# A 16-head masked attention with split operands: a new order of SyncE's queue, and scores eleven slots ahead

## The reference

```
# 1. attention over (2, 8) heads of 768 x 64, masked by a 6-bit hash
mask   = bucket(q @ proj > 0) == bucket(k @ proj > 0)
scores = where(mask, q @ k.T / 8, -1e9)
attn   = exp(scores - max(scores)) / (sum + 1e-9);  x = attn @ v
# 2. x as (2, 768, 512): a causal convolution of 5 taps gives the gate
y = (sigmoid(conv(x)) * (x @ w_val)) @ w_out
# 3. Fourier mixing, norm, feed-forward
u = y + real(fft(fft(y, seq), channels));  un = norm(u)
out = u + relu(un @ w_ch1) @ w_ch2
```

## Time and profile before

| | |
|---|---|
| median of 3 runs | 784.6 us (783.83 to 794.24) |
| the profiled execution, and its span | 781.99 us, span 780.1 us |
| mean granted TensorE clock | 0.954 of full speed |
| TensorE busy | 701.6 us (90%) |
| VectorE busy | 418.7 us (54%) |
| GpSimd busy | 381.9 us (49%) |
| ScalarE busy | 278.4 us (36%) |

### The profile page before, as it was taken

The page is one execution under the profiler, slowest core; times in us unless marked ns, Lnnn a source line. Parts: engine busy times, 40 slices in busy tenths (PEclk is TensorE's granted clock), DMA queues, the critical chain, the costliest instruction groups (busy, mean ns, idle before and its releaser), DMA issues.

```text
span 780.1 us, 10303 instructions
## 1 busy us (share of the span) xinstructions
PE 701.6 (90%) x3696; PEld 647.9 (83%) x3696; DVE 418.7 (54%) x573; ACT 278.4 (36%) x424; POOL 381.9 (49%) x283
## 2 busy tenths in 40 slices
PE   2588889788888879878999999999999999999998
PEld 1388888787878778877989899998999999999897
DVE  3365578778888787797485467942122221212112
ACT  2146564455465454565352444211111111111110
POOL 1047778767878787788286697488100000000000
PEclk9589999999999999997999999999999999999999
DMA  9443645544544635111012112323010000001001
GB/s 246 116 123 98 155 118 139 129 113 107 144 113 112 158 106 129 50 31 42 17 50 61 41 42 75 88 85 95 11 40 0 0 28 13 0 0 41 1 0 41
DMA packets 33608, 57.67 MB, mean 74 GB/s; under 512 B 9232, under 2 KB 15632, under 8 KB 33568
## 3 DMA queue, kind: packets, MB, share of 16 engines
q1 hardware_dynamic: 33568, 57.14, 27.8%
HBM read 31.81 MB, written 3.24 MB: 45 GB/s over the span
## 4 chain that ended last, share of the span: by engine, by line
PE 71%; DVE 17%; DMA 4%; SPq 2%; issue 2%; POOL 2%; ACT 0%; DVEq 0%; POOLq 0%
PE psum L1057 63%; DVE max_col L808 4%; DVE neg_parts L818 2%; DMA a2k<-hash_bits 2%; DVE gate L862 1%; DVE qk_lo L794 1%; POOL p_lo L524 1%; DMA flag_dram<-a2q 1%; PE psum L1133 1%; DVE neg_rest L820 1%; PE psum L1138 1%; PE psum L1139 1%; PE psum L1135 1%; PE psum L1136 1%; DVE gate L859 1%
## 5 line engine op out<-in xcount | busy, mean ns | idle before, releaser
L524 POOL TENSOR_TENSOR p_lo<-probs,p_hi 128x768 fp32r<-128x768 f32 x96 | 190.2, 1996 | 66.4 <-ACT probs L647 65.1
L1028 DVE SCALAR_TENSOR_TENSOR h_lo<-psum,h_hi 128x384 fp32r<-128x384 f32 x64 | 35.7, 558 | 182.7 <-ACT h_hi L769 182.7
L808 DVE TENSOR_REDUCE max_col<-psum 128x1 f32<-128x768 f32 x96 | 91.6, 954 | 76.7 <-PE psum L1057 76.1
L644 ACT ACTIVATE p_hi<-psum 128x768 fp32r<-128x768 f32 x96 | 78.0, 813 | 104.6 <-PE psum L1057 103.0
L769 ACT ACTIVATE h_hi<-psum 128x384 fp32r<-128x384 f32 x64 | 31.5, 492 | 214.5 <-PE psum L1057 214.5
L1057 PE MATMUL psum<-a1k,a1q 128*128 128x384 f32 x192 | 74.2, 386 | 26.8 <-DMA a2k<-hash_bits 17.8
L1057 PE MATMUL psum<-unt_hi,w_hi 128*128 (+1 forms) x256 | 86.9, 339 | 0.0
L1057 PE MATMUL psum<-unt_lo,w_hi 128*128 (+1 forms) x256 | 86.3, 337 | 0.0
L1057 PE MATMUL psum<-unt_hi,w_lo 128*128 (+1 forms) x256 | 85.9, 336 | 0.0
L647 ACT ACTIVATE probs<-psum 128x768 f32<-128x768 f32 x96 | 77.3, 805 | 0.0
L1057 PE MATMUL psum<-w_lo,h_hi 128*128 128x512 f32 x192 | 75.9, 395 | 0.0
(11 more groups left out here) (124 smaller groups left out, 1561.6 us busy)
## 6 DMA issues: line engine op xcount, KB each, us to landing
stg_w<-in_w SPq DMA_DIRECT2D x32, 256.0 KB, 2.6
qk_raw<-in_qk SPq DMA_DIRECT2D x16, 384.0 KB, 5.1
a1k<-qk_hi SPq DMA_DIRECT2D x32, 192.0 KB, 5.1
flag_b<-flag_dram SPq DMA_DIRECT2D x16, 384.0 KB, 3.9
v_raw<-in_v SPq DMA_DIRECT2D x16, 192.0 KB, 3.0
a1q<-qk_hi SPq DMA_DIRECT2D x16, 192.0 KB, 4.7
a2q<-qk_hi SPq DMA_DIRECT2D x16, 192.0 KB, 5.3
a1q<-qk_lo SPq DMA_DIRECT2D x16, 192.0 KB, 5.0
```

The lines of the kernel that those rows point to most:

```text
L524: pool.tensor_tensor(p_lo[i % PBUF][:, :], probs[i % PBUF][:, :], bits(p_hi[i % PHBUF][:, 0:S]), ALU.subtract).then_inc(p_lo_ready, 1)
L644: act.activation(halves(p_hi[i % PHBUF][:, 0:S]), ring[ring_st(i) % 2], ACT.Exp, scale=SCALE).then_inc(p_hi_ready, 1)
L808: dve.tensor_reduce(max_col[:, i % T:i % T + 1], s_ps, AX.XY, ALU.max).then_inc(max_done, 1)
L1028: dve.scalar_tensor_tensor(h_lo[:, half], psum[:, j % 2, 0:HALF], 0.0, bits(h_hi[:, half]), ALU.max, ALU.subtract).then_inc(h_lo_ready, 1)
```

## The change

- `S_LEAD` goes from 10 to 11 and `FIRST` from -20 to -21; the hash, its bits and the loads that belong to it move by a slot, and so does `max_parts` (g modulo 6 from 1 to 0). `turn_max` stays.
- SyncE's loop is reordered. `spread_flag` is cut into `store_flag` (g modulo 6 is 5) and `spread_flag` (1), `spread_rec` into `store_rec` (4) and `spread_rec` (0, for the head before). `load_v` moves from two heads ahead to one, and q and k are loaded at g modulo 12 = 2.
- `scale_x` runs almost a head later, and the taps of the convolution four slots later. At the end of attention four taps move from ahead of the gate products to behind `lo_x(1, c)`, and the last reciprocals ahead of the gate products.
- V is loaded in place, in pieces of 64 columns, into tiles of 128 columns whose other half holds ones; `hi_v` and `lo_v` then work on all 128 columns.
- Units can be weighed unsplit, with two matmuls of probs and v. `SPLIT` lists the tiles of a head that are split; it lists all six.

```diff
-ST_LEAD, S_LEAD = 2, 10
-FIRST = -20
+ST_LEAD, S_LEAD = 2, 11
+FIRST = -21
+
+SPLIT = (0, 1, 2, 3, 4, 5)
+
+def splits_until(i):
+    return i // T * len(SPLIT) + sum(j < i % T for j in SPLIT)
+
+def is_split(i):
+    return i % T in SPLIT
 def hash_slot(pair):
-    return 2 * T * pair - 14
+    return 2 * T * pair - 15
...
             def load_v(n):
+                par = n % 2
                 if n >= 2:
-                    sp.wait_ge(vh_ready, n - 1)
                     sp.wait_ge(vl_ready, n - 1)
-                sp.dma_start(v_raw[n % 2][:, :], v[n // H, n % H, :, :].rearrange("(p t) d -> p (t d)", t=T)).then_inc(v_loaded[n % 2], 16)
+                    sp.wait_ge(pv_done, T * (n - 1))
+                sp.dma_start(tiles(v1[par][:, :])[:, :, par * D:(par + 1) * D],
+                             v[n // H, n % H, :, :].rearrange("(p t) d -> p t d", t=T)).then_inc(v_loaded[par], 16)
...
+            def store_flag(n):
+                sp.wait_ge(max_rows, n + 1)
+                sp.dma_start(flag_dram[n:n + 1, :], bits(a2q[n % SETS][FLAG:FLAG + 1, :])).then_inc(flag_stored[n % 2], 16)
+
             def spread_flag(n):
-                sp.wait_ge(max_rows, n + 1)
-                sp.dma_start(flag_dram[n:n + 1, :], bits(a2q[n % SETS][FLAG:FLAG + 1, :])).then_inc(flag_stored, 16)
...
-            for g in range(FIRST, UNITS + T):
+            for g in range(FIRST, UNITS + 2 * T + 3):
                 pair, n = g // (2 * T), g // T
-                if g % (2 * T) == 10 and 0 <= pair + 3 < NPAIR and pair + 3 >= RAWS // 2:
-                    load_qk(2 * (pair + 3))
-                    load_qk(2 * (pair + 3) + 1)
+                if g % T == 1 and 1 <= n <= NH:
+                    fold_den(n - 1)
+                    if n + 1 < NH:
+                        load_v(n + 1)
+                if g % T == 4 and 1 <= n <= NH:
+                    store_rec(n - 1)
+                if g % T == 0 and 2 <= n <= NH + 1:
+                    spread_rec(n - 2)
                 if g % (2 * T) == 6 and 0 <= pair + 2 < NPAIR:
                     stack(2 * (pair + 2))
                 if g % (2 * T) == 10 and 0 <= pair + 2 < NPAIR:
                     stack(2 * (pair + 2) + 1)
-                if g % (2 * T) == 0 and 0 <= pair + 1 < NPAIR:
-                    stack_bits(pair + 1)
-                if g % T == 2:
-                    if 2 <= n + 2 < NH:
-                        load_v(n + 2)
-                        load_wa(n + 2)
-                    if 1 <= n <= NH:
-                        spread_rec(n - 1)
-                if g % T == 4 and 0 <= n + 1 < NH:
-                    spread_flag(n + 1)
-                if g % T == 1 and 1 <= n <= NH:
-                    fold_den(n - 1)
+                if g % (2 * T) == 11 and 0 <= pair + 2 < NPAIR:
+                    stack_bits(pair + 2)
+                if g % T == 5 and 0 <= n + 1 < NH:
+                    store_flag(n + 1)
+                if g % T == 1 and 0 <= n < NH:
+                    spread_flag(n)
+                if g % (2 * T) == 2 and 2 <= pair + 2 < NPAIR:
+                    load_qk(2 * (pair + 2))
+                    load_qk(2 * (pair + 2) + 1)
+                if g % T == 3 and 2 <= n + 2 < NH:
+                    load_wa(n + 2)
...
-                if g % T == 3 and 0 <= n + 1 < NH:
+                if g % T == 4 and 0 <= n + 1 < NH:
                     lo_v(n + 1)
-                if g % T == 1 and 0 <= n < NH:
+                if g % T == 5 and 0 <= n < NH:
                     split_weights(n)
-                if g % T == 4 and 1 <= n <= NH:
-                    scale_x(n - 1)
-                    pool.wait_ge(x_ready, n)
+                if g % T == 2 and 2 <= n <= NH + 1:
+                    scale_x(n - 2)
+                    pool.wait_ge(x_ready, n - 1)
...
-                if g % T == 1 and 0 <= n + 1 < NH:
+                if g % T == 0 and 0 <= n + 1 < NH:
                     max_parts(n + 1)
-                if g % (2 * T) == 10 and 0 <= pair + 2 < NPAIR:
+                if g % (2 * T) == 9 and 0 <= pair + 2 < NPAIR:
                     sign_bits(pair + 2)
-                if g % (2 * T) == 5 and 0 <= pair + 2 < NPAIR:
+                if g % (2 * T) == 4 and 0 <= pair + 2 < NPAIR:
                     lo_qk(2 * (pair + 2))
-                if g % (2 * T) == 7 and 0 <= pair + 2 < NPAIR:
+                if g % (2 * T) == 6 and 0 <= pair + 2 < NPAIR:
                     lo_qk(2 * (pair + 2) + 1)
-                if g % T == 2 and 1 <= n:
+                if g % T == 3 and 1 <= n:
                     reciprocals(n - 1)
-                slot, tap = (g - 18) // (2 * T), (g - 18) % (2 * T) // 2
-                if 0 <= slot < NPAIR - 1 and (g - 18) % 2 == 0 and tap < KCONV:
+                slot, tap = (g - 22) // (2 * T), (g - 22) % (2 * T) // 2
+                if 0 <= slot and (g - 22) % 2 == 0 and tap < KCONV:
                     convolve(slot, tap)
...
-                if g % (2 * T) == 10 and 0 <= pair + 2 < NPAIR:
+                if g % (2 * T) == 9 and 0 <= pair + 2 < NPAIR:
                     hash_pair(pair + 2)
```

More of the change, by code:

```diff
@@ L57, in hashes_until @@
 def hashes_until(g):
-    return min(NPAIR, max(0, (g + 14) // (2 * T) + 1))
+    return min(NPAIR, max(0, (g + 15) // (2 * T) + 1))
 def sts_until(g):
@@ L203, in build @@
         assert top[0] <= g_at
-        vh = [at(g_at, "vh0", T * P, F32R), after("vh1", T * P, F32R)]
-        vl = [after(f"vl{i}", T * P, F32R) for i in range(2)]
+        vh = [at(g_at, "vh0", len(SPLIT) * P, F32R), after("vh1", len(SPLIT) * P, F32R)]
+        vl = [after(f"vl{i}", len(SPLIT) * P, F32R) for i in range(2)]
         probs_at = top[0]
[L207 to L210, removed]
+        probs = [at(probs_at, "probs0", PCOLS)]
+        probs += [after(f"probs{i}", PCOLS) for i in range(1, PBUF)]
+        p_lo = [at(probs_at, "p_lo0", PCOLS, F32R)]
+        p_lo += [after(f"p_lo{i}", PCOLS, F32R) for i in range(1, PBUF)]
+        top[0] = max(top[0], gv_at)
         sums = [after(f"sums{i}", S) for i in range(2)]
@@ L285, in build @@
         max_rows = sem("max_rows")
[L286 removed]
+        flag_stored = [sem(f"flag_stored{i}") for i in range(2)]
         flag_loaded = [sem(f"flag_loaded{i}") for i in range(2)]
@@ L490, in _ @@
                 pool.memset(bits(p_hi[i][:, S + 1:PCOLS]), 0.0).then_inc(consts_ready, 1)
+            for i in range(PBUF):
+                pool.memset(probs[i][:, S:S + 1], 1.0).then_inc(consts_ready, 1)
+                pool.memset(probs[i][:, S + 1:PCOLS], 0.0).then_inc(consts_ready, 1)
             for par in range(2):
-                own, rest = (slice(D, P), slice(0, D)) if par else (slice(0, D), slice(D, P))
-                pool.memset(bits(tiles(vh[par][:, :])[:, :, rest]), 1.0).then_inc(consts_ready, 1)
-                pool.memset(bits(tiles(vl[par][:, :])[:, :, rest]), 0.0).then_inc(consts_ready, 1)
+                rest = slice(0, D) if par else slice(D, P)
+                pool.memset(tiles(v1[par][:, :])[:, :, rest], 1.0).then_inc(consts_ready, 1)
             pool.wait_ge(consts_ready, CONSTS)
@@ L631, in hi_v @@
                     act.wait_ge(pv_done, T * (n - 1))
-                act.copy(tiles(vh[par][:, :])[:, :, par * D:(par + 1) * D], tiles(v_raw[par][:, :])).then_inc(vh_ready, 1)
+                act.copy(vh[par][:, :].rearrange("p (t d) -> p t d", d=P), split_tiles(v1[par][:, :])).then_inc(vh_ready, 1)
             def rows_of_max(n):
@@ L987, in lo_un @@
                 dve.tensor_tensor(part(unt_lo), tile(psum[:, 6 + t % 2, :]), bits(part(unt_hi)), ALU.subtract).then_inc(unt_lo_ready, 1)
-            for tap in range(3, KCONV):
-                convolve(NPAIR - 2, tap)
+            reciprocals(NH - 1)
             dve.wait_ge(x_ready, NH - 1)
             gate_values(0, 0)
-            reciprocals(NH - 1)
             gate_values(0, 1)
@@ L997, in _ @@
                 lo_x(1, c)
+            for tap in range(1, KCONV):
+                convolve(NPAIR - 2, tap)
             for tap in range(KCONV):
@@ L1125, in weigh_v @@
                 par, w = n % 2, slice(j * P, (j + 1) * P)
-                hi, lo = p_hi[i % PHBUF], p_lo[i % PBUF]
                 first, last = psum[:, PV_BANK, 0:HALF], psum[:, PV_BANK + 1, 0:HALF + 2]
+                start, stop = j == 0, j == T - 1
                 if j == 0:
-                    pe.wait_ge(vl_ready, n + 1)
+                    pe.wait_ge(v_loaded[par], 16 * (n // 2 + 1))
+                    if SPLIT:
+                        pe.wait_ge(vl_ready, n + 1)
                     if n > 0:
@@ L1131, in weigh_v @@
                         pe.wait_ge(sums_ready, n)
-                pe.wait_ge(p_hi_ready, i + 1)
-                pe.matmul(first, vh[par][:, w], hi[:, 0:HALF], start=j == 0, stop=False)
-                pe.matmul(last, vh[par][:, w], hi[:, HALF:PCOLS], start=j == 0, stop=False)
+                if not is_split(i):
+                    pe.wait_ge(probs_ready, i + 1)
```

(17 more changed lines are left out.)

57 lines of the change are left out of this document (33 added, 24 removed).

## The result

The changed kernel takes 828.7 us at the median of four runs, against 784.2 for the one before: a ratio of 1.056 (95% interval 1.050 to 1.0615). The forecast was 788 with 810 as upper end, so the prediction was wrong, on the far side of its range.

A forecast was written before the change was run, and what follows sets the result against it. No engine full: 48.7 us of waits and clock loss in five pairs bound the attention. Attention +1, prologue +1.5, end +1 sum to +3.5 on 782.0, so 785.5; median forecast 788, eight in ten 764 to 810.

The forecast's parts named there:

- SPLIT changes nothing, waits move from the turn to the scores: Attention: every unit keeps six matmuls; the max chain's wait moves from the turn to the scores, growing by 1.8 to 2.0.
- That is 9.8 against 9.7, +0.1 a pair: Attention, per pair of heads: waits and clock loss cost 9.8 us instead of 9.7, +1 us over seven pairs.
- The 1.3 us a pair that the sum kept for the clock: Attention, per pair of heads: loss to a lower clock behind long waits, kept at 1.3 us as before.
- it lies under the chain's 3.6 [...], so I cost it at nothing: Hash bits, second slot of a pair: TensorE's wait of 2.2 us is covered by the max chain's 3.6, cost nothing.
- Wait 3.6 and 4.5 in the chain's slots: Scores wait for the maximum queued behind VectorE's max chain: 3.6 us in one head of a pair, 4.5 in the other.
- the first rival's cheap chain: VectorE's max chain takes 2.0 us because GpSimd, not held for rec_b, is idle: -29 us, 759; chance 17%.
- GpSimd: rec_b's wait goes, the wider lo_v is covered: GpSimd in attention: 25.3 us of waiting for rec_b go and pay for lo_v's +0.85 a head, 14 us in all.
- The V load in pieces of 256 B: V load one head ahead: landing was 3.0 us, some 8 available; even doubled to 6 it is covered, so nothing.
- Prologue +1.5: Before the first PV: one more scores-only slot costs 0.7 to 2.70 us, taken as +1.5.
- End of attention +1: Last slots, where GpSimd sets the pace: scale_x, lo_v and last weight split less rec_b's wait, +1 us, between -3 and +4.
- the moved taps: Four taps behind the gates (6.2 us) run into an idle 3.92; the 2.3 left over are covered by matmuls.
- the third: SyncE's queue: store_rec behind reciprocals delays stack and bits 2 us a pair beyond cover: +14, 802; chance 12%.

The follow-up runs named there:

- e1: The changed kernel with the weight split back at slot 1 of a head on GpSimd: 780.5 us, ratio 0.9926 to the kernel before.
- e7: e1 with the flag stored and spread in one step at slot 4, ahead of the hash bits in SyncE's queue: 811.3 us, ratio 1.0331.
- e4: e1 with max_col in two halves and the max chain behind the next slot's maximum (slot 1 instead of 0): 801.7 us, ratio 1.0175.
- e5: e1 with scores ten slots ahead again, and max chain, hash, q/k splits and bits on their old slots: 812.1 us, ratio 1.0361.
- e8: e1 with hi_v and lo_v again on the own 64 columns of each tile only: four runs of 797.7 to 811.0 us.
- e10: e1 with convolution taps and second qk_lo moved away from the max chain, and hi_v and lo_v on the own 64 columns only: 780.9 us, ratio 0.9972.
- e11: e1 with one more wait of SyncE, for the p_lo of slot 5, ahead of each weight load: 803.1 us, ratio 1.0251.
- e2: The changed kernel, split still at slot 5, with the weight load asked for at slot 1 of the head after: 795.4 us, ratio 1.0109.

## Why the prediction was wrong, step by step

- **SPLIT changes nothing, waits move from the turn to the scores:** right. neg_parts 23.1 to 2.8 us, max_col 25.6.
- **"That is 9.8 against 9.7, +0.1 a pair": the step that failed.** It was (236.9 - 163.2) / 5 = 14.7 us a pair. The sum had a term for each engine's edits, but for SyncE's queue it began at sign_bits' end and listed store_rec, stack and bits. `load_wa` stands ahead of store_rec in that list, and its wait for a split that was moved from slot 1 to 5 was not read. The bits' wait at m1 came out at up to 7.1 us instead of 2.2. With that term gone (e1) it is 203.8 us for the five pairs, 8.1 a pair. The 1.3 us a pair that the sum kept for the clock were too few as well: after the bits' wait in slot 37 the granted clock was 0.50 from 202.4 to 207 us, some 2.3 us of work lost in that one place.
- **"it lies under the chain's 3.6 [...], so I cost it at nothing":** wrong as a habit. It nearly held in e1, where the bits' waits are 1.4 to 1.7 us. But e7's 3.4 us more in the queue took the cover away, and they passed through to TensorE, six times.
- **Wait 3.6 and 4.5 in the chain's slots:** the size is near. In e1 slots 37 and 38 (m1, m2) took 4.16 and 4.10, 3.3 over two free ones, and slots 42 to 44 had 4.4 over three. But the judgement that this order makes it worse than the order before fell with e4 and e5. Its estimate took one length for the chain, 4.35. In e1 the chain takes 4.8 us where it begins in m0 and 2.25 in m6, as GpSimd's operations fall. In the changed kernel it takes 2.6 and 2.1 to 2.6 from slot 24 to 72: the first rival's cheap chain (2.0) was nearly there, and gave nothing while the bits were late.
- **GpSimd: rec_b's wait goes, the wider lo_v is covered:** wrong in the changed kernel (32.0 us of waiting), since rec_dram is behind the same stop; in e1 the wait in all is 10.6. The wider lo_v costs nothing; the narrow one does (e8, e10). The V load in pieces of 256 B landed in 3.1 us, before 3.0. The line rate that the Trainium skill ("DMA: Bandwidth & Descriptors", Specifications) puts at 512 B and more made no difference that this trace shows.
- **Prologue +1.5:** it was +4.8, and +3.9 in e1, both beyond the 2.70 that I took as the most. The slot itself cost that price: e1's first PV comes 2.7 us behind that of e5, which has one such slot fewer. The other 1.2 us of e1, which e5 has too, are not explained.
- **End of attention +1:** the slots from 72 on lost 9.1 us, with the stand, and 5.2 in e1 without it, so the +1 was too small and its bound of +4 too; 4.0 of the 5.2 are in slots 72 to 84. Behind PV it was 0.3, so the moved taps were covered as said.
- **Rivals:** the third, that SyncE's new order only changes what it stands for, had the right place, but named reciprocals instead of the split and allowed +14.

## What to carry to other kernels

When an instruction moves, look for every queue that waits for it, and list the waits of an in-order queue in the order in which they are met. Here a wait at slot 3 for work at slot 5, for a weight load that was wanted only two heads later, cost 23 to 25 us alone (e11) and 47 to 50 with the late split itself, through the bits issued behind it. Cost a wait in a queue by what stands behind it, not by what it guards. And take the largest wait away before judging the rest: the same move of taps gave 14 us with the queue free and nothing with it blocked.

## What was not expected of the hardware

Less work on an engine made the kernel slower (e8: GpSimd's lo_v 0.85 us shorter a head, at least 17 us more in all). VectorE's operations of 0.17 us took up to 1.85 beside GpSimd's (e2), and which engine waits can hang on a difference of some tenths of a microsecond in when they are ready. The pattern then repeats from pair to pair, since the slots of both engines are tied to each other: the five chains of e1 that begin in m0 took 4.78, 4.78, 4.79, 4.79 and 4.79 us. So a small shift is not averaged out but multiplied by the number of pairs.

A long wait also costs more than its length, because the granted clock falls while TensorE stands: in e7 TensorE is idle from 187.3 to 193.0 us, and the clock is 1.00 until 189 and 0.50 from 190. These are the 3.1 us right behind a wait, in the changed kernel (6.04 us for the bits), e7 (5.75 for the bits), e5 (3.88 for neg_parts) and e8 (3.88 for max_col), and last in e1 (1.39 for max_col):

```profile
202.40:205.50 3.10, 3.09 (x10) 3.09 (x11) 0.96 (x1) 0.00 (x0) 0.43 (x1) 0.50 0.62 155
193.00:196.10 3.10, 3.08 (x10) 3.08 (x11) 0.96 (x1) 0.00 (x0) 1.16 (x1) 0.50 0.96 262
287.40:290.50 3.10, 3.05 (x13) 2.86 (x14) 1.69 (x2) 1.42 (x2) 0.00 (x0) 0.50 0.02 5
234.40:237.50 3.10, 3.06 (x10) 3.07 (x10) 1.38 (x2) 0.00 (x0) 0.78 (x1) 0.50 0.46 178
222.00:225.10 3.10, 3.07 (x20) 2.70 (x21) 2.06 (x2) 0.77 (x2) 2.61 (x2) 1.00 0.85 233
```

At 0.50, that is 1.2 of 2.4 GHz, TensorE got through 10 matmuls (13 where six of them were the turn's tiny ones), at 1.00 through 20. That is a good part of what e5, e7 and e8 cost beyond their longer waits. Over slots 12 to 72 the clock's mean was 0.89, 0.90 and 0.91 in them, and 0.97 in e1. No run here holds the clock fixed, so the two parts are read from traces and not from an experiment.
